# Two of the first weight-split subtractions moved from VectorE to GpSimd, with ScalarE scaling their input in place

## The reference

```python
for t in range(S):                                   # B, H, S, D = 4, 8, 768, 48
    cur = einsum('bhd,bhe->bhde', u * k[t], v[t])
    y[t] = einsum('bhd,bhde->bhe', r[t], state + cur)
    state = w[t][..., None] * state + einsum('bhd,bhe->bhde', k[t], v[t])
...
h = x @ w_in                                         # [3072, 384] @ [384, 2048]
g = maximum(h, 0) + alpha * minimum(h, 0)
x = g @ w_out                                        # [3072, 2048] @ [2048, 384]
...
expert = argmax(x @ w_gate)                          # 8 experts, top 1
out = gate * (maximum(x @ w1[expert], 0) @ w2[expert])
```

## Time and profile before

| | us |
|---|---|
| median of 3 runs | 776.35 |
| lowest, highest | 773.27, 780.42 |
| time of the profiled execution | 781.25 |
| its span, first to last instruction | 779.5 |
| busy: TensorE, VectorE, ScalarE, GpSimd | 733.1, 475.7, 365.6, 392.9 |
| mean granted TensorE clock | 0.987 of full speed |

### The profile page before, as it was taken

One profiled execution on the slowest core, in us unless ns is written; L12 is line 12 of the kernel. 1 busy time (PEld: TensorE's weight loads), 2 busy tenths in 40 slices (PEclk: granted clock), 3 DMA queues, 4 the chain that ended last, 5 costly groups with the idle time before them and its releaser, 6 DMA issues.

```text
span 779.5 us, 17757 instructions
## 1 busy us (share of the span) xinstructions
PE 733.1 (94%) x6779; PEld 516.6 (66%) x6779; DVE 475.7 (61%) x967; ACT 365.6 (47%) x735; POOL 392.9 (50%) x372
## 2 busy tenths in 40 slices
PE   4699999999989999999999999998999999999995
PEld 4466656656655665665666666556688878788783
DVE  6998898779666878776787864645333333333331
ACT  3652577656655756746756665542122212212210
POOL 5445488769668869778777876252111111111111
PEclk9998999999999999999999999999999999999998
DMA  9835636365364653645545247994699866766763
GB/s 341 324 150 185 209 132 244 105 241 174 131 238 179 234 215 121 233 165 172 201 142 187 82 162 243 341 345 158 225 383 395 294 245 214 254 237 219 265 222 116
DMA packets 42694, 170.04 MB, mean 218 GB/s; under 512 B 5198, under 2 KB 13136, under 8 KB 37104
## 3 DMA queue, kind: packets, MB, share of 16 engines
q1 hardware_dynamic: 30160, 108.18, 39.1%
q10 hardware_dynamic: 8928, 50.51, 18.5%
q0 software_dynamic: 3520, 10.17, 3.3%
HBM read 132.30 MB, written 37.33 MB: 218 GB/s over the span
## 4 chain that ended last, share of the span: by engine, by line
PE 60%; POOL 9%; DMA 9%; DVE 6%; issue 6%; ACT 3%; SPq 1%; ACTq 0%; POOLq 0%; DVEq 0%
PE bank L1733 5%; PE bank L1876 5%; PE bank L1878 5%; PE bank L1877 5%; PE bank L1735 4%; PE bank L1734 4%; PE bank L1724 4%; PE bank L1722 4%; PE bank L1721 4%; PE bank L1842 4%; PE bank L1844 4%; PE bank L1843 4%; DMA arena<-w_exp_dram 3%; POOL act_buf L606 3%; DMA route_rows<-xrow,pos 2%
## 5 line engine op out<-in xcount | busy, mean ns | idle before, releaser
L606 POOL TENSOR_TENSOR act_buf<-act_buf 128x384 f16<-128x384 f32 x128 | 120.2, 939 | 139.8 <-ACT act_buf L809 138.8
L1291 DVE SCALAR_TENSOR_TENSOR act_buf<-neg,slope,bank 128x384 f32<-128x384 f32 x128 | 77.7, 607 | 92.1 <-ACT neg L802 91.4
L692 POOL DMA_INDIRECT out_dram<-neg,dest x28 | 27.5, 984 | 201.7 <-DVE neg L1560 194.2
L1733 PE MATMUL bank<-arena,act_buf 128*128 128x392 f16 x384 | 127.2, 331 | 1.6 <-ACT xrow L765 1.4
L1721 PE MATMUL bank<-xh,arena 128*128 128x384 f16 x384 | 125.5, 327 | 2.2 <-DVE xl L1093 1.5
L1734 PE MATMUL bank<-arena,act_buf 128*128 128x392 f16 x384 | 127.1, 331 | 0.0
L1735 PE MATMUL bank<-arena,act_buf 128*128 128x392 f16 x384 | 127.0, 331 | 0.0
L1722 PE MATMUL bank<-xl,arena 128*128 128x384 f16 x384 | 125.3, 327 | 0.0
L1842 PE MATMUL bank<-shared,arena 128*128 128x128 f16 x672 | 114.1, 219 | 1.9 <-DVE shared L1486 1.7
L1844 PE MATMUL bank<-shared,arena 128*128 128x128 f16 x672 | 114.1, 219 | 0.0
L1843 PE MATMUL bank<-shared,arena 128*128 128x128 f16 x672 | 114.1, 219 | 0.0
(11 more groups left out here) (185 smaller groups left out, 1563.9 us busy)
## 6 DMA issues: line engine op xcount, KB each, us to landing
arena<-expert_split ACTq DMA_DIRECT2D x28, 1536.0 KB, 7.5
arena<-w_exp_dram SPq DMA_DIRECT2D x32, 768.0 KB, 6.3
expert_split<-arena SPq DMA_DIRECT2D x32, 768.0 KB, 4.7
arena<-expert_split SPq DMA_DIRECT2D x9, 1536.0 KB, 9.2
arena<-rk_in_dram SPq DMA_DIRECT2D x24, 512.0 KB, 6.0
arena<-rk_tok_dram SPq DMA_DIRECT2D x24, 384.0 KB, 3.3
arena<-w_dram SPq DMA_DIRECT2D x24, 256.0 KB, 6.8
shared<-route_rows ACTq DMA_DIRECT2D x31, 197.0 KB, 2.5
```

The costliest lines, as they stand in the source:

```text
L606: pool.tensor_tensor(gl[:, f % 4, :], gf[:, f % 4, :], gh[:, f % 4, :], ALU.subtract).then_inc(gl_done, 1)
L1733: pe.matmul(at, gh[:, f % 4, ts], woh[:, f, :], start=(f == 0), stop=False)
```

## The change

The second quarter of `w_out` and the third quarter of `w_in` get their low parts on GpSimd. GpSimd's step is a plain `tensor_tensor` subtract without a scale, so ScalarE first writes the scaled float32 value over the input, in place, and then copies that to the float16 high part. The other quarter of each half is scaled and rounded in one pass as before. So ScalarE's pass of 3072 elements becomes three of 1536 for each of the two halves. GpSimd's two steps stand at f = 2, behind `hidden_low` and ahead of `row_weights`, and at f = 4, behind `hidden_low` and ahead of `decayed_k`. VectorE's steps at f = 4 and f = 5 go; of the half of `w_in`, `w_in_low(1, 1)` stays at f = 6. New semaphores `w_out_lo1` and `w_in_lo2` take their place in the waits of TensorE and in the wait of SyncE's load of `w_out` half 1.

```diff
--- before.py
+++ after.py
@@ -250,6 +250,10 @@
         dve_const = sem("dve_const")
         pads_out = sem("pads_out")
         w_arrived = [sem(f"w_arrived{i}") for i in range(2)]
+        w_out_scaled = sem("w_out_scaled")
+        w_out_lo1 = sem("w_out_lo1")
+        w_in_scaled = sem("w_in_scaled")
+        w_in_lo2 = sem("w_in_lo2")
         w_third_in = sem("w_third_in")
         rk_arrived = [sem(f"rk_arrived{i}") for i in range(2)]
         v_in = [sem(f"v_in{i}") for i in range(NC)]
@@ -431,7 +435,8 @@
             load_tok(0, 1, 1)
             load_v(0, 1, 1)
             load_w(0, 1, 2)
-            sp.wait_ge(w_out_ready, 3)
+            sp.wait_ge(w_out_ready, 2)
+            sp.wait_ge(w_out_lo1, 1)
             sp.dma_start(wide[3], w_out[1]).then_inc(wide_in[3], 16)
             load_v(0, 1, 2)
             load_rk(0, 1, 2)
@@ -600,6 +605,17 @@
                 pool.tensor_tensor(split[:, i, 1, s], stage[:, i, s], split[:, i, 0, s], ALU.subtract
                                    ).then_inc(unit_lo, 1)
 
+            def w_out_low1():
+                pool.wait_ge(hi_done, 2)
+                pool.tensor_tensor(wol[:, 4:8, 0:DM], wide[3].rearrange("p (f n) -> p f n", n=DM)[:, 4:8, :],
+                                   woh[:, 4:8, 0:DM], ALU.subtract).then_inc(w_out_lo1, 1)
+
+            def w_in_low2():
+                fs = slice(0, FF // 4)
+                pool.wait_ge(hi_done, 4)
+                pool.tensor_tensor(first_w_in(1, wil)[:, :, fs], wide[4].rearrange("p (k n) -> p k n", k=KD)[:, :, fs],
+                                   first_w_in(1, wih)[:, :, fs], ALU.subtract).then_inc(w_in_lo2, 1)
+
             def hidden_low(g, f):
 
                 pool.wait_ge(gh_done, NF * g + f + 1)
@@ -633,6 +649,10 @@
                         if g >= 2 and not end and f == 0:
                             unit_low(unit - 2)
                         if start:
+                            if f == 2:
+                                w_out_low1()
+                            if f == 4:
+                                w_in_low2()
                             if f == 1:
                                 row_products(nb, nh, 0)
                             if f == 2:
@@ -791,6 +811,24 @@
                 act.activation(first_w_in(i, wih), wide[at].rearrange("p (k n) -> p k n", k=KD), ACT.Copy, scale=WIS
                                ).then_inc(hi_done, 1)
 
+            def first_w_out_high():
+
+                half = lambda i: wide[3].rearrange("p (f n) -> p f n", n=DM)[:, 4 * i:4 * i + 4, :]
+                act.wait_ge(wide_in[3], 16)
+                act.activation(woh[:, 0:4, 0:DM], half(0), ACT.Copy, scale=WOS)
+                act.activation(half(1), half(1), ACT.Copy, scale=WOS).then_inc(w_out_scaled, 1)
+                act.wait_ge(w_out_scaled, 1)
+                act.activation(woh[:, 4:8, 0:DM], half(1), ACT.Copy).then_inc(hi_done, 1)
+
+            def later_w_in_high():
+
+                quarter = lambda tile, i: tile.rearrange("p (k n) -> p k n", k=KD)[:, :, i * FF // 4:(i + 1) * FF // 4]
+                act.wait_ge(wide_in[4], 16)
+                act.activation(quarter(wide[4], 0), quarter(wide[4], 0), ACT.Copy, scale=WIS).then_inc(w_in_scaled, 1)
+                act.activation(first_w_in(1, wih)[:, :, FF // 4:FF // 2], quarter(wide[4], 1), ACT.Copy, scale=WIS)
+                act.wait_ge(w_in_scaled, 1)
+                act.activation(first_w_in(1, wih)[:, :, 0:FF // 4], quarter(wide[4], 0), ACT.Copy).then_inc(hi_done, 1)
+
             def w_out_high(i):
                 act.wait_ge(wide_in[3], 16 * (i + 1))
                 act.activation(woh[:, 8 * i:8 * i + 8, 0:DM], wide[3].rearrange("p (f n) -> p f n", n=DM),
@@ -878,7 +916,7 @@
             att_high(0, 0, 2, 1, b_y)
             turned_k(0, 0, 2, b_o[1])
             turned_x(0, 0, 1, b_o[2])
-            w_out_high(0)
+            first_w_out_high()
             turned_x(0, 0, 2, b_o[2])
             gate_cols_copy(1)
             gate_cols_high(0, b_gt[:, 0:8 * NE])
@@ -902,7 +940,7 @@
                         if start and f == 0:
                             decayed_keys(0, 1, 0)
                         if start and f == 1:
-                            w_in_high(1)
+                            later_w_in_high()
                             v_high(0, 1, 0)
                         if not end:
                             c = (f - 3) // 4
@@ -1342,10 +1380,8 @@
                             decays(b + 1, half, 0, b_hid[f][:, 0:C])
                         if f == 12:
                             decays(b + 1, half, 1, b_hid[f][:, 0:C])
-                    if start and f == 4:
-                        w_out_low(0, 1)
-                    if start and f in (5, 6):
-                        w_in_low(1, f - 5)
+                    if start and f == 6:
+                        w_in_low(1, 1)
                     if start and f in (9, 11):
                         w_out_low(1, f // 11)
                     if start and f == 13:
@@ -1707,8 +1743,10 @@
                     pe.wait_ge(wide_free[0], 2)
                 if first and f == 5:
                     pe.wait_ge(late_copied, 1)
-                if first and f in (8, 12):
-                    pe.wait_ge(wide_free[1], f // 4 - 1)
+                if first and f == 8:
+                    pe.wait_ge(w_in_lo2, 1)
+                if first and f == 12:
+                    pe.wait_ge(wide_free[1], 1)
                 if not (first and TILE_BEFORE[f] < 0):
                     pe.wait_ge(g_done, UP + NF * g + TILE_BEFORE[f] + 1)
                 if f == 0 and not first and not last_half:
@@ -1784,11 +1822,13 @@
                             rank(g - 1)
                         elif f in (13, 15):
                             turn(f // 15)
-                        if start and f in (0, 4):
-                            pe.wait_ge(w_out_ready, 2 + f // 4)
+                        if start and f == 0:
+                            pe.wait_ge(w_out_ready, 2)
+                        if start and f == 4:
+                            pe.wait_ge(w_out_lo1, 1)
                         if start and f in (8, 12):
                             pe.wait_ge(wide_free[0], 1 + f // 4)
-                            pe.wait_ge(w_out_ready, 4)
+                            pe.wait_ge(w_out_ready, 3)
                         outputs(g, f)
 
             pe.wait_ge(pool_const, 3)
```

## The result

| | before | after |
|---|---|---|
| median of 20 runs | 775.83 us | 782.09 us |
| profiled execution, its span | 781.25, 779.5 | 781.07, 779.3 |

The ratio is 1.0072 (95% interval 1.0058 to 1.0087): the change costs 5.6 us (4.5 to 6.8). The forecast was +3.0.

The account below looks back on a forecast made before the run. TensorE was taken as the bound, busy 63.90 of 68 us in the first group. With w_out at 0 and +3.0 us from w_in, term 1's +1.1 included, 776.35 + 3.0 = 779.3 us; range 775 to 783.5.

Parts of the forecast that it names:

- the chain that the forecast calls decisive: GpSimd's w_in subtract delays decayed_k, then decayed_keys, neg and gf of tile 6, and the scores of chunk 1: +3.0 us.
- the forecast's own signs of being wrong: Subtracts under 2 us, scores of chunk 1 starting no later than before, or the clock falling in the new wait.
- w_out passes: ScalarE at 35.22: one pass of 2.77 us becomes three taking 4.4 us; cover 1.3 us, so no cost.
- term 1: ScalarE's three w_in passes at 49.00 delay neg and gf, so the gate products start late: +1.1 us, bounds 0 and +1.8.
- term 2: GpSimd's w_out subtract, 3.1 us ahead of row_weights, delays row_sums and low_k; cover 0.3 us, so 0, at most +1.0.
- term 3: GpSimd's w_in subtract ahead of decayed_k delays the scores of chunk 1: +3.0 us including term 1, bounds +1.9 and +5.0.
- rival 3: New wait before the scores brings TensorE to 1.2 GHz: 5 us on top of +3.0, 784.4 us; chance 0.10.
- wait before the state product: TensorE's 1.64 us wait at 84.40: TensorE and the chain both move by 3.0, so it neither covers nor adds.
- Rivals 1 and 2: Relief counts, cost covered: 775.5 us, chance 0.10; 3 us swallowed later or subtracts much quicker: 776.4 us, chance 0.12.
- Rival 4: The forecast's mechanism at its upper bound, +4 to +6, two subtracts at 3.7 to 4.4 us; inside the forecast's 0.68.

Follow-up runs that it names:

- w_out_only: The change's w_out part alone, three ScalarE passes and GpSimd's subtract at f = 2, w_in as before; ratio 1.0004.
- pad_small: The kernel before plus an unread ScalarE step of 192 elements ahead of the w_in pass at f = 1; ratio 1.0007.
- passes_only: The kernel before with ScalarE's w_in pass at f = 1 made into the change's three, low parts still on VectorE; ratio 1.0028, +2.2 us.
- subtract_early: The change with GpSimd's w_in subtract moved ahead of hidden_low(4), into GpSimd's idle time; ratio 1.0033, +2.6 us.
- both_moved: The change with ScalarE's w_in passes moved to f = 4 and both GpSimd subtracts moved ahead of hidden_low(4); ratio 0.9996.
- passes_late: The change with ScalarE's three w_in passes moved from f = 1 to f = 4, subtracts unmoved; ratio 1.0029, +2.3 us.
- pad_middle: The kernel before plus an unread ScalarE step of 1152 elements ahead of the w_in pass at f = 1; ratio 1.0038, +2.9 us.
- w_in_only: The change's w_in part alone, w_out's low part staying on VectorE and its ScalarE pass staying one; ratio 1.0078, 6.1 us.
- w_in_again: The change's w_in part alone, profiled once more without timed runs; low stretch 6.8 us, scores 3.6 us late.
- gate_mixed: The kernel before with the three parts of outputs(1) placed between TensorE's late gate products; ratio 0.9983.

## Why the prediction was right, and where its sum was short

The range and the direction held (at most 1%, slower), and so did the chain that the forecast calls decisive; 5.6 us is nearly twice the 3.0 of the sum. That it stayed inside the range is owed to the range's width and not to the sum, which had no term for 2 of the 5.6 us. One of the forecast's own signs of being wrong appeared too: the clock fell behind the new wait. By its steps, from the common point:

| step | forecast | measured |
|---|---|---|
| w_out passes, cover 1.3 us | 0 | 0 (`w_out_only`) |
| term 1, gate products late | +1.1 | +1.1 |
| term 2, w_out subtract, 3.1 us, cover 0.3 us | 0 | 0, 3.09 us long, cover 2.3 us |
| term 3 without term 1 | +1.9 | +2.4 |
| low stretch at the gate products | not in the sum | +1.8 |
| second low stretch, behind the scores | rival 3, up to +5 | +0.3 |
| wait before the state product | follows | shrank, 1.64 to 0.45 |

*Term 1* was right to 0.05 us, cover included (`pad_small`, `passes_only`). *Term 2* was right, but its cover in the change was not the forecast's 0.3: `low_k` ended at 61.95 and TensorE, held up by its low clock, came for it at 64.21.

*Term 3* was mis-sized by 0.5 us. The `gf` of tile 6 came at 31.52 from the common point in place of 26.86, +4.66: 2.88 from the passes and the clock (`passes_only`), and 1.8, which is the forecast's 75.4 for that step less term 1. That is luck in part: the subtract took 3.41 us in place of 3.1, and `decayed_k` behind it 1.29 in place of 1.61. The 0.5 comes behind that step: `gate_cols_low` (L1119), 64 elements and 0.20 us before, took 0.80 at 74.70, while `decayed_q` (L566) ran on GpSimd from 74.23 to 75.41. Both its inputs are in SBUF, and it ended 0.1 us after GpSimd's step. The change brought the two steps together; `subtract_early` has 0.79 there too, and its relief is 0.4 us where the wait had 0.80 to give. The step before and in `subtract_early`:

```profile
74.27 0.20 DVE L1081 SCALAR_TENSOR_TENSOR arena<-xrow,arena 128x64 f16<-128x64 f32 x1
```

```profile
71.91 0.79 DVE L1119 SCALAR_TENSOR_TENSOR arena<-xrow,arena 128x64 f16<-128x64 f32 x1
```

By the Trainium skill's "SBUF — State Buffer", section "SBUF: two separate sides", the two shut one another out for a whole instruction; the rows agree, but no run took this meeting alone apart.

*The missing term* is the clock at the gate products. The 6.8 us of low clock stood in the profile of before (0.95 over 43 to 111), and I asked only whether the new wait before the scores would make another. That rival was right in its mechanism and wrong in its price: the fall came behind the wait of 3.18 us, lasted 3.4 us and cost 0.3 us, since the wait before the state product covered the rest (it fell from 1.64 to 0.45). The costly place was the one where TensorE had no slack and the clock fell in the kernel before too. `passes_only` gives it by itself: 2.87 us late at the scores with 1.11 us of delay, so 1.76 us for 3.4 us more at half clock (half of 3.4 is 1.7).

Rivals 1 and 2 are out: with the subtract in GpSimd's idle time the first came true in part (`both_moved`), but at 0.4 us, not 0.8. Rival 4 (+4 to +6) has the measured number but not its reason: it wants subtracts of 3.7 to 4.4 us, and they took 3.1 and 3.4. The measured steps, 1.11 + 1.76 + 2.38 + 0.27 = 5.5 us, are by their making the delay of the state product in one profile; what bears them out is `passes_late`, where the third stands alone at 2.41, and the 5.6 us timed. The timed runs of the two halves, 2.2 (`passes_only`) and 2.3 (`passes_late`), add to 4.5, each with an interval of 1.3 to 1.5 us to either side.

Still open is why the low stretch takes 6.8, 10.2 or 13.6 us in a given execution, and by how much its mean grows; passes_only's 2.2 us (0.9 to 3.5) is the best measure of the two together.

## What to carry to other kernels

A helper engine's idle time is worth something only if the new step is written ahead of the wait that makes it; written behind, it stood whole on the chain with its 3.4 us, although its input was 17 us old. Before costing a delay of TensorE, look at the granted clock where it falls: beside a stretch at half clock, 0.7 us of delay went with 2.4 us at the scores (`pad_middle`). And a step taken off an engine is worth what TensorE waited for it (at most 0.8 us here, in fact 0.4), not its length (twice 1.75).

## What the runs showed of the hardware

TensorE's clock fell to 1.2 GHz while the profile had it busy without a gap, in 48 matmuls of 8 columns, in all twelve profiles with these in their old order; 1.5 us of dense matmuls mixed in did not prevent it. A wait of 3.2 us before the scores brought it down for 3.4 us in all five profiles that had one (the change twice, `passes_late`, `w_in_only`, `w_in_again`); a wait of 1.6 us before the state product left it at 1.00 in eight profiles and was followed by a fall in one (`gate_mixed`). ScalarE took 1.47 us for 1536 elements to float32 in place and the same to float16. GpSimd took 3.09 us for 1536 elements, and 3.41 and 3.28 where a VectorE step with both inputs in SBUF was still running as it began (in the change from 65.47 to 66.73, in `subtract_early` from 59.60 to 60.22).
